# Attention and two mixtures of experts on one core: overflow lists made between the first experts' products, first w1 loaded during attention, second logits laid out by partition

## What is computed

```python
# q, k, v: (4, 8, 768, 64); x: (3072, 512); w1: (8, 512, 1024); w2: (8, 1024, 512)
x = attention(q, k, v, n_global=8, n_local=96)
...
do_compute = x @ w_skip > 0
logits = x[do_compute] @ w_gate
e_idx = argmax(logits, 1)
for e in range(8):                       # first mixture: y = x + gate * expert(x)
    h = maximum(xc[e_idx == e] @ w1[e], 0)
    out[e_idx == e] += gate_w * (h @ w2[e])
...
for idx in argsort(-(x @ w_gate2).flatten()):   # second mixture: 384 tokens each
    assign token idx // 8 to expert idx % 8 unless assigned or full
out[mask_e] = maximum(x[mask_e] @ w1b[e], 0) @ w2b[e]
```

## Time and profile before

| | |
|---|---|
| runs shown | 894.22, 897.20, 899.83 us, median 897.2 |
| profiled execution | 898.36 us, span 896.6 us |
| TensorE busy | 765.6 us (85%) |
| VectorE busy | 537.9 us (60%) |
| ScalarE busy | 458.2 us (51%) |
| GpSimd busy | 165.3 us (18%) |
| mean granted clock of TensorE | 0.938 |
| moved by DMA | 157.93 MB, mean 176 GB/s |

### The profile page before, as it was taken

How to read it: one execution, slowest core, us unless ns; L and a number is a source line. 1 busy time by engine, 2 the same in 40 slices (tenths; PEclk the granted TensorE clock), 3 DMA queues, 4 the chain that set the end, 5 groups by cost and what they waited for, 6 DMA issues and landing times. The chain is left out here.

```text
span 896.6 us, 15433 instructions
## 1 busy us (share of the span) xinstructions
PE 765.6 (85%) x5529; PEld 696.5 (78%) x5529; DVE 537.9 (60%) x1431; ACT 458.2 (51%) x919; POOL 165.3 (18%) x186
## 2 busy tenths in 40 slices
PE   0899999999549898999999712999999999999994
PEld 0899999999449796999999612878788788788893
DVE  3977777776456755665566248474766656574410
ACT  2788888897234542554455102535353545445350
POOL 5000000000021121122211111131313141423321
PEclk9999999999769999999999755999999999999998
DMA  8888999993674436344653004666776757679751
GB/s 180 178 197 228 244 216 276 207 279 83 218 244 180 138 125 228 127 159 172 211 206 113 6 5 149 168 211 142 236 165 211 188 168 186 186 181 287 203 107 38
DMA packets 68985, 157.93 MB, mean 176 GB/s; under 512 B 14230, under 2 KB 17558, under 8 KB 68896
## 3 DMA queue, kind: packets, MB, share of 16 engines
q1 hardware_dynamic: 57184, 121.05, 46.3%
q0 software_dynamic: 11712, 35.73, 16.5%
HBM read 119.11 MB, written 23.50 MB: 159 GB/s over the span
## 5 line engine op out<-in xcount | busy, mean ns | idle before, releaser
L1581 PE MATMUL r_ph<-r_xh,r_w1h 128*128 128x384 f32 x256 | 92.4, 361 | 0.0
L549 ACT ACTIVATE pr<-pr,nmx 128x232 f32<-128x232 f32 (+1 forms) x192 | 79.9, 467 | 17.3 <-DVE nmx L645 17.3
L1581 PE MATMUL r_ph<-r_xh,r_w1l 128*128 128x384 f32 x256 | 88.3, 345 | 0.0
L1581 PE MATMUL r_ph<-r_xl,r_w1h 128*128 128x384 f32 x256 | 87.8, 343 | 0.0
L977 PE MATMUL m_ph<-m_xh,m_w1h 128*128 128x256 f32 (+1 forms) x288 | 84.8, 295 | 0.0
L1102 ACT ACTIVATE m_hh<-m_ph 128x256 fp32r<-128x256 f32 (+1 forms) x72 | 26.8, 372 | 112.1 <-PE m_ph L977 107.6
L977 PE MATMUL m_ph<-m_xh,m_w1l 128*128 128x256 f32 (+1 forms) x288 | 82.8, 287 | 0.0
L977 PE MATMUL m_ph<-m_xl,m_w1h 128*128 128x256 f32 (+1 forms) x288 | 82.6, 287 | 0.0
L422 PE MATMUL sc<-kk,qh 128*128 128x256 f32 x192 | 59.2, 329 | 23.9 <-DVE ql L623 23.9
L1595 PE MATMUL r_py<-r_w2h,r_hh 128*128 128x512 f32 x192 | 76.5, 399 | 0.0
L645 DVE CUSTOM_DVE_ANT_0 pr<-sc,bias 128x232 f32<-128x232 f32 (+1 forms) x192 | 64.9, 374 | 19.1 <-PE sc L423 18.6
(11 more groups left out here) (267 smaller groups left out, 1984.4 us busy)
## 6 DMA issues: line engine op xcount, KB each, us to landing
m_w<-moe_w SPq DMA_DIRECT2D x36, 512.0 KB, 5.5
row_buf<-moe_w SPq DMA_DIRECT2D x9, 2048.0 KB, 8.4
r_w<-moe_w SPq DMA_DIRECT2D x32, 512.0 KB, 5.7
r_w<-moe_w SPq DMA_DIRECT2D x8, 2048.0 KB
r_w2l<-r_w POOLq DMA_DIRECT2D x32, 512.0 KB, 5.4
k_raw<-kI SPq DMA_DIRECT2D x32, 416.0 KB, 8.2
q_raw<-qT SPq DMA_DIRECT2D x32, 384.0 KB, 9.3
x_rows<-row_buf SPq DMA_DIRECT2D x8, 1536.0 KB, 9.0
```

The costliest lines, as they stand in the source:

```text
L549: nc.scalar.activation(pr[n % PRS][:, t, lo:CW], pr[n % PRS][:, t, lo:CW], ACT.Exp, bias=nmx[n % PRS][:, t:t + 1], scale=-1.0).then_inc(ex ...
L1581: last = nc.tensor.matmul(ph[m % 4][:, 0:CAP], w[:, c, m * P:(m + 1) * P], x[:, c, :], start=(c == 0 and a == 0), stop=(c == KC - 1 and a ...
```

## The change

- `w1`'s buffer is taken ahead of attention, and `load_w1`, four loads, is called for expert 0 behind the last v loads of attention; the first mixture starts without it. For k of 1 and more the loads wait as before.
- `load1(1, 1)` (with all that follows in SP's queue) now also waits for the first gather.
- `count_extra` runs in block 1, `table_extra` in block 2, each on VectorE between the w2 split of m = 0 and the low part of m = 1, instead of behind the block.
- `z_dram` is (128, 24, 8), by partition, so its store and its load are one piece of 768 B for each partition instead of 24 of 32 B. The scatters write the same rows of 32 B at other row numbers, `zrows1`, which VectorE makes with `z_rows_of` (five instructions) in `gate_of_tokens` and in `list_extra`. The first scatter of logits also waits for `gated`.
- In overflow blocks from the second on, which this input does not need, GpSimd copies one more column.

```diff
@@ -149,7 +149,13 @@
         xb = [row_buf[:, s * QT_N * DM:(s + 1) * QT_N * DM].rearrange("p (i d) -> p i d", d=DM) for s in range(2)]
+        w1 = late.enter_context(nc.sbuf_tensor("m1_w1", [P, KC, F], F32))
         stored = late.enter_context(nc.semaphore("x_stored"))
+        w1_loaded = [late.enter_context(nc.semaphore(f"m1_w1_loaded{c}")) for c in range(KC)]
+
+        def load_w1(sp, e):
+            for c in range(KC):
+                sp.dma_start(w1[:, c, :], w1a[bass.ds(e, 1), c * P:(c + 1) * P, :].rearrange("o p n -> p (o n)")).then_inc(w1_loaded[c], 16)
 
@@ -336,6 +342,7 @@
                     load_v(PAIRS - 1)
+                    load_w1(sp, 0)
                     store(B - 1)
@@ -740,7 +748,7 @@
 
-            w1, w2 = tb("w1", [P, KC, F]), row_buf[:, 0:FC * DM].rearrange("p (c n) -> p c n", n=DM)
+            w2 = row_buf[:, 0:FC * DM].rearrange("p (c n) -> p c n", n=DM)
             w1h, w1l = (tb(f"w1{x}", [P, KC, F], F32R) for x in "hl")
@@ -775,14 +783,15 @@
 
-            row1, row_ready = tb("row1", [P, 1], I32), sem("row_ready")
+            row1, zrow1, row_ready = tb("row1", [P, 1], I32), tb("zrow1", [P, 1], I32), sem("row_ready")
+            zrows1 = tb("zrows1", [P, SLOTS + OVER + 2], I32)
+            base, lanes = (tb(x, [P, OVER + 2]) for x in ("base", "lanes"))
             z_stored, cleared, chain = sem("z_stored"), sem("cleared"), sem("chain")
...
             passed = [sem(f"passed{i}") for i in range(5)]
-            w1_loaded = [sem(f"w1_loaded{c}") for c in range(KC)]
             w2_loaded, w1_high, w1_low, w2_high, w2_low = (sem(x) for x in ("w2_loaded", "w1_high", "w1_low", "w2_high", "w2_low"))
@@ -827,11 +836,9 @@
                 def load1(k, e):
-                    if not isinstance(k, int) or k:
-                        sp.wait_ge(w1_high, KC * k)
-                        sp.wait_ge(w1_low, KC * k)
-                    for c in range(KC):
-                        sp.dma_start(w1[:, c, :], w1a[bass.ds(e, 1), c * P:(c + 1) * P, :].rearrange("o p n -> p (o n)")).then_inc(w1_loaded[c], 16)
+                    sp.wait_ge(w1_high, KC * k)
+                    sp.wait_ge(w1_low, KC * k)
+                    load_w1(sp, e)
 
@@ -839,10 +846,10 @@
 
-                load1(0, 0)
-                sp.dma_start(z_dram.rearrange("(t p) e -> p t e", p=P), logits[:, :, E + 1:]).then_inc(z_stored, 16)
+                sp.dma_start(z_dram, logits[:, :, E + 1:]).then_inc(z_stored, 16)
                 sp.wait_ge(stored, 32 * B)
                 load2(0, 0)
+                sp.wait_ge(gathered[0], moved(0))
                 for k in range(1, E):
@@ -863,15 +870,21 @@
 
+                z_rows = z_dram.rearrange("p t e -> (p t) e")
+
                 def rows_at(k, t):
                     return row1[:] if not isinstance(k, int) else rows1[:, column_of(k, t)]
+
+                def z_rows_at(k, t):
+                    return zrow1[:] if not isinstance(k, int) else zrows1[:, column_of(k, t)]
 
...
                         g.tensor_copy(row1[:], rows1[:, column_of(k, 0)]).then_inc(row_ready, 1)
-                        pool.wait_ge(row_ready, k - E)
+                        g.tensor_copy(zrow1[:], zrows1[:, column_of(k, 0)]).then_inc(row_ready, 1)
+                        pool.wait_ge(row_ready, 2 * (k - E))
                     elif k >= 2:
@@ -888,9 +901,11 @@
                     pool.wait_ge(z_kept, k + 1)
+                    if isinstance(k, int) and k == 0:
+                        pool.wait_ge(gated, 1)
                     settle(pool, passed[1])
                     for t in tiles(k):
-                        g.indirect_dma_start(z_dram, bass.IndirectOffsetOnAxis(ap=rows_at(k, t), axis=0), zo[s][:, t, :], None,
+                        g.indirect_dma_start(z_rows, bass.IndirectOffsetOnAxis(ap=z_rows_at(k, t), axis=0), zo[s][:, t, :], None,
                                              bounds_check=N - 1, oob_is_err=False).then_inc(z_scattered[s], 16)
@@ -1171,6 +1186,10 @@
                     for m in range(FC):
+                        if isinstance(k, int) and m == 1 and k == OVER_AT - 1:
+                            count_extra()
+                        if isinstance(k, int) and m == 1 and k == OVER_AT:
+                            table_extra()
                         dve.wait_ge(h_high, FC * k + m + 1)
@@ -1201,6 +1220,14 @@
                     return v.tensor_tensor(out, parts[:, 0:cols], found[:, 0:cols], ALU.add)
+
+                def z_rows_of(parts, cols, out):
+
+                    link(v.tensor_scalar(lanes[:, 0:cols], parts[:, 0:cols], 1.0, float(NT), ALU.subtract, ALU.mult))
+                    link(v.tensor_scalar(base[:, 0:cols], parts[:, cols:2 * cols], 1.0 / P, None, ALU.mult))
+                    link(v.tensor_tensor(lanes[:, 0:cols], lanes[:, 0:cols], base[:, 0:cols], ALU.add))
+                    link(v.tensor_scalar(base[:, 0:cols], parts[:, 0:cols], 0.0, float(2 * NO_ROW), ALU.is_equal, ALU.mult))
+                    return v.tensor_tensor(out, lanes[:, 0:cols], base[:, 0:cols], ALU.add)
 
@@ -1237,6 +1264,7 @@
 
+                    link(z_rows_of(row_parts, SLOTS, zrows1[:, 0:SLOTS]))
                     dve.wait_ge(exped, 1)
@@ -1294,6 +1322,7 @@
                     link(gates_from(over_parts[:, 2 * W:], W, gates1[:, SLOTS:]))
+                    link(z_rows_of(over_parts, W, zrows1[:, SLOTS:]))
                     rows_of(over_parts, W, rows1[:, SLOTS:]).then_inc(over_listed, 1)
@@ -1306,10 +1335,6 @@
                     one_block(k, BLK)
-                    if k == 1:
-                        count_extra()
-                    if k == OVER_AT:
-                        table_extra()
                     next_parts(k + 1, (k + 1) % 2, BLK)
@@ -1450,7 +1475,7 @@
 
-                sp.dma_start(logits2[:], z_dram.rearrange("(t p) e -> p t e", p=P)).then_inc(z_loaded, 16)
+                sp.dma_start(logits2[:], z_dram).then_inc(z_loaded, 16)
                 for k in WINDOWS:
@@ -2080,7 +2105,7 @@
     x1_dram = nc.dram_tensor("x1_rows", (N, DM), F32).ap()
-    z_dram = nc.dram_tensor("gate2_logits", (N, E), F32).ap()
+    z_dram = nc.dram_tensor("gate2_logits", (P, NT, E), F32).ap()
     build(nc, t["qT"], t["kT"], t["kI"], t["vL"], t["vG"], t["n_global"], t["n_local"], t["w_gate1"], t["moe_w1"], t["moe_w2"],
```

## The result

The changed kernel takes 885.68 us (median of four runs, 884.23 to 890.38), the kernel before 898.31 us in the runs beside it; the ratio is 0.9856, with a 95% interval of 0.9828 to 0.9884. That is 12.6 us less by the two medians and 12.9 by the ratio. The forecast was 885.3, out of a sum of -12.45. The profiled execution has a span of 883.7 us against 896.6, so the two traces can be set against each other stretch by stretch.

The account below looks back on a forecast made before the run. TensorE sets the middle stage's pace, held up by VectorE's late low parts and, at the opening, by late gathered rows. -9.05 - 3.4 = -12.45 us gave 885.9 or 884.7; forecast 885.3, range 881.5 to 890.5.

Parts of the forecast that it names:

- Part 1: Blocks 1 and 2: moving overflow work into the products removes two TensorE waits with slow tails; -9.05 us.
- 31.6 over block 2: Sign to look for: SP's loads of w2 31.6 us apart over block 2, against 36.05 before.
- I price no slow tail: At m=5 of blocks 1 and 2: new waits of 0.7 and 0.2 us, no cost for a lowered clock behind them.
- Part 2: Five small VectorE instructions after the first lists and five after the overflow lists: cost nothing; 2.2 us without cover.
- Parts 3 and 4: Mixture's opening: early first w1 and held-back second w1 give the gathers a quieter DMA; rows at 255.1, -3.4 us.
- Part 5: Logits by partition: store falls to 128 pieces, counted in the opening; faster load before second routing worth 0, hidden by fills.
- B: Opening: gathers as late as now, set by GpSimd's issue and scattered rows' latency; costs 3.4 us, 888.7; chance 0.14.
- C: Blocks 1 and 2: VectorE and GpSimd block each other during gather issue; 4.4 us of wait at m=5, 889.7; chance 0.09.
- D: TensorE waits at m=5 as long as it did at the turns; only the 3.4 us stay, 894; chance 0.03.
- cover of 5.44 us: Block 2: from split start to m=5's first product, 5.44 us in which TensorE's four banks hide VectorE's moved work.
- E: Block 0: the clock does not come back, TensorE's work of 264 to 288 takes twice its 24 us; 909, chance 0.02.
- F: More gain than forecast: rows at 253.3 and no wait at m=5; 882.6 or lower, chance 0.06.

Follow-up runs that it names:

- the packed store: Changed kernel with ScalarE first copying the second gate's logits into a tile without gaps, so the store has no small packets; one run, 884.32 us.
- the kernel that splits in attention: Changed kernel with all four ScalarE and VectorE parts of the first w1's split done in attention's last steps; ratio 0.9852 to the kernel before.
- the doubled work: Changed kernel with count_extra done twice in its new place in block 1; ratio 0.9965 to the kernel before.
- the last version: Changed kernel with count_extra in two halves, three of four first-w1 splits in attention, second routing started after 8 of 17 fills; 881.43 us, ratio 0.9801.

## Why the prediction was right, point by point

**The sum.** The forecast was nearer than its terms. Of the -12.45 us, -9.05 and -3.4, the traces gave -7.77 - 3.63 = -11.40. The other 1.5 us of the 12.9 lie in four stretches for which the sum had nothing (-0.42, -0.30, -0.36 and -0.42 in the table); only the 0.30 belong to the change, by the clock that came back a little sooner. That the total came out within half a microsecond is luck; the mechanisms were right, except where a part below says so.

**Part 1, the move.** The sum had -9.05 us for three spacings, and they gave -7.77. Two of its terms were right to 0.3 us. The removed wait and tail of block 1 with `table_extra`'s new wait were -5.33 + 0.2 and came to 31.35 to 26.37, -4.98. `count_extra`'s new wait was 0.7 and is 0.69 us; the spacing grew by 0.94. VectorE's timeline of the changed kernel shows the steps of that sum, split, moved work (18 instructions, first and last), low part:

```profile
286.29 0.69 DVE L1197 TENSOR_TENSOR m_w2l<-row_buf,m_w2h 128x512 fp32r<-128x512 f32 x1
286.90 0.33 DVE L1289 TENSOR_TENSOR m_extra<-m_incl,sizes 128x176 f32<-128x176 f32 x1
...
291.78 0.18 DVE L1308 SCALAR_TENSOR_TENSOR m_col<-m_total,m_away 128x24 bf16<-128x24 f32 x1
292.00 0.42 DVE L1194 SCALAR_TENSOR_TENSOR m_hl<-m_ph,m_hh 128x256 fp32r<-128x256 f32 x1
```

The term that was off is the third. I had -4.62 for block 2's wait and tail, with "The 5.41 us of overflow products stay where they are", and it came to -3.73. They do stay, and take 5.42 us, but the clock now falls within them, which it did not in the kernel before, and the first products of block 3 run at the lower level: 32.32 - 26.02 - 5.42 = 0.88 us. So the sign "31.6 over block 2" came out at 32.3, and there is a stretch at 0.50 there. The step that failed is "I price no slow tail": it looked for a fall behind waits only. In 13 of the 14 traces, all but that of the kernel before, the clock falls in or right behind these products. One execution of each kernel was profiled, so whether that is the kernel or the execution can't be told. But that the clock can fall without a wait could be read from the kernel before. In its overflow block, in the products of 128 columns, TensorE is busy without a gap and the clock falls at 496, as it does in that block in all 14 traces (columns: PE busy, granted clock, DMA share, GB/s):

```profile
494.00:496.00 2.00, 2.00 (x20) 1.00 0.04 8
496.00:498.00 2.00, 2.00 (x13) 0.54 0.00 0
...
502.00:504.00 2.00, 2.00 (x8) 0.75 0.00 0
```

**Part 2, the index arithmetic.** Costed at nothing, and nothing is seen: five instructions of 0.16 to 0.17 us at 258.03 to 259.02, and five of 0.18 us before block 3, with no wait of TensorE behind either.

**Parts 3 and 4, the opening.** -3.4 us expected, -3.63 measured; the rows are in 3.9 us after the second gather's issue instead of the 4.15 that I took. w2, which I left at 242.99, is issued at 241.87 and has landed by 250.2, not 251.4. The mechanism was right too: a busy DMA made the rows late. Putting back w1 costs 2.82 us, putting back the second expert's early load 1.39. Nothing waits for that load now that it comes later. Of what stood ahead of w2, "and (part 5) no small pieces" was wrong.

**Part 5, the logits.** "The store falls from 3072 pieces to 128 of 768 B" is false, and so is what the list of changes says of the store; I looked at the destination and not at the source. It cost the forecast nothing, because w1 was what had pushed the store and w2 into the gathers, and the packed store shows that the small pieces are worth nothing once w1 is gone. The load did change, 1.9 us to landing instead of 3.4, and gave nothing, as forecast: GpSimd's fills hold the routing.

**The rivals.** B (the gathers as late as now) had half a point: the slow issue is real and lies in VectorE's splits, but it costs 1.3 us (1.5 in the kernel that splits in attention), and the traffic's 3.6 us are beside it. C (VectorE and GpSimd block each other inside the moved work) did not happen: issues of 1.10 and 1.01 us. D did not, by the cover of 5.44 us, which the doubled work confirms. E did not: the clock was back at 259.3, 4.9 us after the first transposes, where it took 5.6 before, which goes with the 0.30 us in the table's third row. F's extra gain, without the wait at m=5, is what the last version takes.

## What to carry to other kernels

Work that holds up a split at a block's end can be hidden inside the block, up to what the banks let the products run ahead; count that cover from the trace (5.44 us here), since beyond it every microsecond counts once, and again in the clock that falls behind it. A gather of scattered rows wants no bulk load beside it: load the first weights where DMA is idle, and hold the next ones back until the rows are in. Count the pieces of a DMA on both sides: a contiguous destination changes nothing while the source has gaps, and the profile's count of small packets tells which transfer changed.

## What the runs showed of the hardware that I had not expected

- The granted clock can fall while TensorE is busy without a gap: in the 24 overflow products of 120 columns, 0.225 us apart, it went from 1.00 to 0.50 some 4 us after they began, in two places of the program, and it cost 0.9 us; in the other traces with the moved work the spacing over them is 0.8 to 2.1 us longer than the products alone make it. In the overflow block, whose products have 128 columns, it fell in all 14 traces. In the kernel before, the 24 products ran at 1.00 throughout. That they followed there some 4 us behind the end of an earlier fall doesn't explain it, as they did so in the kernel with all but the move too, and there the clock fell. Why it didn't in the one trace stays open.
- The tail behind a wait is not in proportion to it: 1.6 to 1.8 us behind waits of 3.0 and 3.5 us, 4.3 us behind one of 5.72 us, with the clock at 0.50 for some 10 us instead of 3.4.
- A split put on VectorE at attention's end costs more than its own delay: behind a wait of TensorE of 2.46 us the clock fell at 233.6, ahead of the last twelve products, and they took 2.82 us; behind 1.33 us, in the last version, it was 233.5 and 2.71 us; behind 1.07 us, in the changed kernel, 235.4 and 1.55 us.
- GpSimd's issue of a gather takes 2.27 and 1.70 us beside VectorE's splits of 1024 columns, and 1.28 and 1.00 us without them.
